# Keys and values in rings: the 24 V rows that two neighbouring tiles share are copied by ScalarE from one ring place to the next, for tiles 2 to 6 of each batch

## The chip, the cores and the metric

The program runs on one core of a Trainium2 chip. What counts is the device time of one execution in microseconds (us). The names of the engines are those of the profile: PE is TensorE, ACT is ScalarE, DVE is VectorE, POOL is GpSimd, SP is SyncE, which only issues DMAs here. A name with a q (SPq, ACTq) is that engine's instruction queue issuing a DMA.

## The reference

Chunked attention, then a soft mixture of experts, then a routed one. All data is float32.

```python
# attention: 4 batches, 8 heads, 768 tokens, head size 64, 8 memory tokens
for c in range(nc):                      # chunks of 32 queries
    l_start = max(0, c_start - 16)       # 16 tokens to the left
    r_end = min(S, c_end + 8)            # 8 tokens to the right
    k_full = np.concatenate([mem_k, k[:, :, l_start:r_end]], axis=2)
    v_full = np.concatenate([mem_v, v[:, :, l_start:r_end]], axis=2)
    scores = scale * np.matmul(q_c, k_full.transpose(0, 1, 3, 2))
    a = softmax(scores)
    out[:, :, c_start:c_end] = np.matmul(a, v_full)
# soft mixture: 3072 tokens, 512 wide, 8 experts x 4 slots, hidden 1024
logits = x @ phi; slot_input = softmax(logits, axis=0).T @ x
slot_out[e] = relu(slot_input[e] @ w1[e]) @ w2[e]
x = softmax(logits, axis=1) @ slot_out
# routed mixture: each token goes to one of 8 experts
out[mask] = gate * relu(x[mask] @ w1[e]) @ w2[e]
```

## The kernel before

**Tiles.** A tile is 96 query tokens (three chunks) of one batch with all 8 heads; a batch has 8 tiles, the program 32. A tile's keys and values are 120 token rows (96 with 16 to the left and 8 to the right) and 8 memory rows, 128 partitions in all. Neighbouring tiles overlap by 24 rows. The first tile of a batch starts at token 0 and the last ends at token 767, so there the overlap lies at other rows; for tiles 2 to 6 of a batch the first 24 rows of a tile are rows 96 to 119 of the tile to its left.

**Loads.** `k_in`, `q_in` and `v_in` are rings of four places each. SP runs through the tiles: in its round t it issues K (L399), the memory rows of K in the first two tiles of a batch (L401), Q (L403), and then V of tile t-4 (L410) with the memory rows of V (L412) for the first four tiles of a batch. A row of one head is 64 numbers, a packet of 256 bytes, so 96 rows are 768 packets and 120 rows are 960. K is loaded with 96 rows only, since ACT copies the overlap of the transposed keys inside SBUF (L1286). V was loaded with all 120. Before K of tile t SP waits until tile t-4 has been transposed (`kq_turned`); before V of tile t until tile t-4 has been weighted (`weighted`). `v_arrived[r]` counts the landings of place r, V and memory rows alike.

**The pipeline.** PE, ACT, DVE and POOL each run an instruction list written by hand, step j = 0 to 39, with the tiles staggered. On PE step j holds: transposes of the probabilities of tile j-4 (L625), scores of tile j-1 (L608; in every fourth step these two change places), transposes of K and Q of tile j (L644, L647), transposes of x of tile j-5 (L655), and last the product of V and probabilities of tile j-4 (L686), before which PE waits for V to have landed. On ACT step j holds: two copies of the transposed probabilities (L1258, L1263), the exponential of tile j-2 (L1251), copies of transposed Q and K of tile j (L1276, L1286, L1287), and last, once PE has done L686 of tile j-4, the copy of its result (L1298). POOL subtracts the row maximum (L549) and multiplies by the inverse row sum (L544). After four tiles come a few instructions more for the first router.

**Weights.** ACT issues one load of a 2 MB expert matrix every four steps (L1320, then L1326), after L1298, seven in all. When the last tiles of attention release their places, SP issues the other matrices in quarters (L434, each behind a wait for PE) and then whole (L499).

**After attention.** The first mixture (PE L750, L774), routing, then for half of the span the second mixture, in which PE is busy without a gap (L906, L916).

Of the kernel before, what the change touches and what calls it, by code (L numbers as in the profile page):

```python
# [24 lines left out]
def build(nc, q, k, v, mem_k, mem_v, phi, w1m, w2m, w_gate, w_ogate, w1, w2, out, rows_dram, g_dram):  # L25
    B, H, S, D = q.shape
    MEM = mem_k.shape[2]
    CHUNK, LEFT, RIGHT = 32, 16, 8
    CH = 3
    TQ = CH * CHUNK  # L30
# [21 lines left out]
    KQV = 4  # L52
# [30 lines left out]
    with ExitStack() as ctx:  # L83
# [3 lines left out]
        def sem(name):  # L87
            return ctx.enter_context(nc.semaphore(name))
# [128 lines left out]
        small_in = sem("small_in")  # L217
        kq_in = [sem(f"kq_in{i}") for i in range(KQV)]
        v_arrived = [sem(f"v_arrived{i}") for i in range(KQV)]
        kq_turned = sem("kq_turned")  # L220
        kt_copied = sem("kt_copied")
        qt_copied = sem("qt_copied")
# [116 lines left out]
        def k_rows(t):  # L339
# [2 lines left out]
            first = ends[t % TPB - 1] if t % TPB else 0  # L342
            return first, ends[t % TPB] - first

        def kq_landings(b, t):

            both = 48 if t % KQV < 2 else 32
            per_batch = both + 32 * (TPB // KQV - 1)
            uses = t // TPB * per_batch + both + t % TPB // KQV * 32
            return uses if b is None else b * per_batch + uses  # L350
# [9 lines left out]
        def quad_end(b, t):  # L360

            return live(b, t) and t % 4 == 3
# [9 lines left out]
        def heads(ap):  # L372
            return ap.rearrange("p (h d) -> p h d", h=H)
# [19 lines left out]
        def _(sp):  # L393
# [11 lines left out]
            def load_v(b, t, batch):  # L405

                r = t % KQV
                start = min(max(TQ * (t % TPB) - LEFT, 0), S - CTX)
                until(sp, weighted, b, t - KQV + 1)
                sp.dma_start(heads(v_in[0:CTX, r, :]), v_bs[batch, start:start + CTX]).then_inc(v_arrived[r], 16)  # L410
                if t % TPB < KQV:
                    sp.dma_start(heads(v_in[CTX:NK, r, :]), mv_bs[batch]).then_inc(v_arrived[r], 16)  # L412

# [182 lines left out]
        def _(pe):  # L596
# [32 lines left out]
            def step(b, j):  # L629
# [46 lines left out]
                if live(b, j - 4):  # L676

                    pe.wait_ge(v_arrived[(j - 4) % KQV], landings(b, j - 4, 16))
                    until(pe, pt_copied_low, b, j - 3)
                    until(pe, pt_copied_high, b, j - 3)  # L680
                    until(pe, xt_copied, b, j - 4)
# [561 lines left out]
        def _(act):  # L1243
# [21 lines left out]
            def step(b, j):  # L1265
# [27 lines left out]
                if live(b, j - 4):  # L1293

                    until(act, weighted, b, j - 3)
                    until(act, x_turned, b, j - 3 - XT)
                    quads_done(act, logit_made, b, j - 5)
                    sc.copy(x_t[:, (j - 4) % XT].rearrange("p c t -> p (c t)"), bank[6][:, 0:KD * TQ]).then_inc(xt_copied, 1)  # L1298
                if quad_end(b, j - 6):

                    g = (j - 6) // 4 if b is None else b * QPB + (j - 6) // 4
# [183 lines left out]
```

## Time and profile before

| | us |
|---|---|
| median of 3 runs | 486.86 (484.9 to 488.0) |
| profiled execution, its own time | 486.13 |
| its span, first to last instruction | 483.9 |
| PE busy | 447.3 (92%) |
| ACT busy | 269.1 (56%) |
| DVE busy | 214.4 (44%) |
| POOL busy | 179.6 (37%) |

The busy shares are means over stages that differ. Attention fills the span up to about 171 us, the first mixture with the routing lasts until about 243 us, and the rest is the second mixture. The line of the DMA shows 16 engines busy at 90% or more in nearly every slice up to 210 us, and at a tenth or less in most of the last 170 us. The line of bytes per second shows that the same busy engines move 160 to 280 GB/s during attention, and 420 GB/s after it.

### The profile page before, as it was taken

What the parts mean: (1) busy time and instruction counts of PE and PEld (TensorE: products, weight loads), DVE (VectorE), ACT (ScalarE), POOL (GpSimd) and SP (SyncE); (2) the same over time, 40 slices, a digit from 0 to 9 for tenths busy, and PEclk for the clock granted to TensorE, in tenths of its full rate; (3) what the DMA queues carried; (4) which work ended last, traced back from release to release, by engine and by line L of the source; (5) the groups of instructions that cost most, each with busy time, mean ns of one, the idle gap of its engine ahead of it and who ended that gap; (6) DMA issues with size and microseconds to landing.
All of it is one profiled execution on the core that took longest, in us unless ns stands there. A gap on an engine that the chain in (4) does not pass through costs nothing.

```text
span 483.9 us, 13207 instructions
## 1 busy us (share of the span) xinstructions
PE 447.3 (92%) x4708; PEld 251.3 (52%) x4709; DVE 214.4 (44%) x927; ACT 269.1 (56%) x465; POOL 179.6 (37%) x145
## 2 busy tenths in 40 slices
PE   4599999788999799998999999999999999999992
PEld 3488778577877653365554434443444344434430
DVE  2898988786899563019722112121212121212110
ACT  1587787575877520104164567665666566656540
POOL 2788887685888401000250122231223122101110
PEclk9999999998999999999999999999999999999998
DMA  9999999999999989999996976610011101000000
GB/s 156 192 262 234 234 275 215 225 272 184 281 241 273 372 315 336 427 429 420 420 389 221 407 279 238 219 45 25 23 46 39 31 23 46 32 34 22 24 0 0
DMA packets 98618, 95.63 MB, mean 198 GB/s; under 512 B 86664, under 2 KB 87096, under 8 KB 95896
## 3 DMA queue, kind: packets, MB, share of 16 engines
q1 hardware_dynamic: 93544, 73.18, 55.4%
q10 hardware_dynamic: 1792, 14.88, 8.2%
q0 software_dynamic: 3248, 7.14, 4.2%
q8 instruction: 19, 0.31, 0.3%
q14 instruction: 15, 0.12, 0.1%
HBM read 88.49 MB, written 7.74 MB: 199 GB/s over the span
## 4 chain that ended last, share of the span: by engine, by line
PE 66%; DVE 11%; SPq 10%; issue 4%; DMA 3%; POOL 3%; ACT 1%; DVEq 0%; ACTq 0%; POOLq 0%
PE bank L906 40%; PE bank L886 6%; DVE arena L1034 3%; PE bank L774 3%; SPq L410 3%; SPq L412 3%; SPq L399 2%; DMA arena<-in_mem_v_dram 2%; PE bank L625 2%; DVE row_sum L1053 2%; PE bank L831 2%; PE bank L686 2%; PE bank L608 2%; PE bank L703 1%; PE bank L750 1%
## 5 line engine op out<-in xcount | busy, mean ns | idle before, releaser
L916 PE MATMUL bank<-arena 128*64 128x512 f32 x448 | 196.5, 595 | 0.0
L906 PE MATMUL bank<-arena 128*64 (+1 forms) x448 | 196.5, 595 | 0.0
L906 PEld LDWEIGHTS bank<-arena 128*64 128x64 f32 x448 | 59.7, 137 | 119.9 <-issue 119.5
L1165 DVE TENSOR_SCALAR arena<-bank 128x256 f32<-128x256 f32 x112 | 39.7, 417 | 168.3 <-PE bank L886 96.4
L578 POOL DMA_INDIRECT out_dram<-arena,tok_sorted x28 | 28.3, 1010 | 177.0 <-ACT arena L1373 177.0
L549 POOL TENSOR_TENSOR arena<-arena,row_max 96x1024 f32<-96x1024 f32 x32 | 60.6, 1893 | 21.7 <-DVE row_max L1034 21.6
L544 POOL TENSOR_TENSOR arena<-arena,row_inv 96x1024 f32<-96x1024 f32 x32 | 60.6, 1894 | 17.5 <-DVE row_inv L1022 17.5
L1034 DVE CUSTOM_DVE_ANT_0 arena<-bank,masks 96x128 f32<-96x128 f32 x256 | 56.5, 282 | 15.0 <-issue 15.0
L1373 ACT ACTIVATE arena<-bank,gate_sorted 128x512 f32<-128x512 f32 x28 | 19.2, 687 | 75.3 <-PE bank L916 75.1
L916 PEld LDWEIGHTS bank<-arena 128*64 128x64 f32 x448 | 59.8, 137 | 0.0
L1393 ACT COPY arena<-arena 128x2048 f32 x27 | 51.3, 1898 | 3.2 <-DVE half_expert L1204 2.3
L1398 ACT COPY arena<-arena 128x2048 f32 x27 | 51.2, 1895 | 0.5 <-issue 0.4
L572 POOL DMA_INDIRECT arena<-rows_scratch,row_sorted x27 | 26.2, 970 | 61.8 <-DVE row_sorted L1193 53.9
L608 PE MATMUL bank<-arena 64*96 64x128 f32 x512 | 37.6, 288 | 5.6 <-ACT arena L1287 3.7
L1251 ACT ACTIVATE arena<-arena 96x1024 f32<-96x1024 f32 x32 | 34.0, 1062 | 12.7 <-POOL arena L549 12.5
L1053 DVE TENSOR_REDUCE row_sum<-arena 96x8 f32<-96x1024 f32 x32 | 38.6, 1206 | 0.7 <-ACT arena L1251 0.7
L608 PEld LDWEIGHTS bank<-arena 64*96 64x96 f32 x512 | 30.5, 167 | 14.2 <-ACT arena L1287 6.6
L686 PE MATMUL bank<-shared,arena 128*64 128x96 f32 x512 | 28.2, 252 | 8.6 <-DMA arena<-in_mem_v_dram 2.8
L625 PE MATMUL bank<-ident,arena 96*128 96x96 f32 x256 | 28.7, 256 | 1.7 <-DVE hid_rows_a L1059 1.0
L686 PEld LDWEIGHTS bank<-shared,arena 128*64 128x64 f32 x512 | 22.3, 137 | 14.6 <-issue 6.9
L625 PEld LDWEIGHTS bank<-ident,arena 96*128 96x128 f32 x256 | 22.8, 143 | 6.1 <-DVE hid_rows_a L1059 1.3
L1298 ACT COPY token_side<-bank 128x384 f32<-128x384 f32 x32 | 15.3, 478 | 18.1 <-PE bank L686 17.7
(189 smaller groups left out, 546.5 us busy)
## 6 DMA issues: line engine op xcount, KB each, us to landing
arena<-in_moe_w_dram SPq DMA_DIRECT2D x18, 2048.0 KB, 9.9
arena<-in_moe_w_dram ACTq DMA_DIRECT2D x7, 2048.0 KB, 9.4
arena<-in_moe_w_dram SPq DMA_DIRECT2D x24, 512.0 KB, 7.7
arena<-in_v_dram SPq DMA_DIRECT2D x32, 240.0 KB
arena<-in_q_dram SPq DMA_DIRECT2D x31, 192.0 KB, 5.0
arena<-in_k_dram SPq DMA_DIRECT2D x20, 192.0 KB, 4.5
arena<-in_moe_w_dram SPq DMA_DIRECT2D x2, 1024.0 KB, 9.2
arena<-in_k_dram SPq DMA_DIRECT2D x4, 240.0 KB
```

The lines of the kernel that those rows point to most:

```text
L544: g.tensor_tensor(probs[:, t % 4], probs[:, t % 4], row_inv[:, t % 2, :].unsqueeze(2).to_broadcast([TQ, H, NK]), ALU.mult).then_inc(p_norm ...
L549: g.tensor_tensor(probs[:, t % 4], probs[:, t % 4], row_max[:, t % 2, :].unsqueeze(2).to_broadcast([TQ, H, NK]), ALU.subtract).then_inc(sh ...
L608: ins = mm(bank[2 + h % 2][0:TQ, (h // 2) * NK:(h // 2 + 1) * NK], q_t[lo:lo + D, (j - 1) % 2, h // 2, :], k_t[lo:lo + D, (j - 1) % 2, h / ...
L625: ins = nc.tensor.transpose(bank[4 + h // 4][:, (h % 4) * TQ:(h % 4 + 1) * TQ], probs[:, (j - 4) % 4, h, :], ident[0:TQ, 0:TQ])
L686: ins = mm(bank[6][lo:lo + D, (h // 2) * TQ:(h // 2 + 1) * TQ], v_in[:, (j - 4) % KQV, h * D:(h + 1) * D], p_t[:, (j - 4) % 2, h, :], star ...
L906: mm(bank[4 + par][0:HR, :], h_t[:, par, lo:lo + HR], w2_all[:, bass.ds(at_w2 * SEG + f * DM, DM)], start=(f == 0), stop=(f == KF - 1))
L916: ins = mm(bank[4 + par][HR:TR, :], h_t[:, par, lo + HR:lo + TR], w, start=(f == 0), stop=(f == KF - 1))
L1034: ins = vec.tensor_tensor_reduce(out=probs[:, (j - 1) % 4, h, :], in0=bank[2 + h % 2][0:TQ, (h // 2) * NK:(h // 2 + 1) * NK], in1=masks[:, ...
L1053: vec.tensor_reduce(row_sum[:, j % 2, :], probs[:, (j - 2) % 4], AX.X, ALU.add).then_inc(row_summed, 1)
L1165: ins = vec.tensor_scalar(h_t[:, j % 2, 2 * r * 128:(2 * r + 2) * 128].rearrange("p (c a t) -> p a c t", c=2, a=2), bank[r][:, j % 2 * 256 ...
L1393: sc.copy(w2_second[j % 2][:, 0:SEG // 2], w2_all[:, bass.ds(e * SEG, SEG // 2)]).then_inc(second_low, 1)
L1398: sc.copy(w2_second[j % 2][:, SEG // 2:SEG], w2_all[:, bass.ds(e * SEG + SEG // 2, SEG // 2)]).then_inc(second_high, 1)
```

## The change

V of tiles 2 to 6 of a batch is loaded with its last 96 rows only. The 24 rows before them are copied inside SBUF by ACT from the place of the tile to the left: partitions 96 to 119 of one ring place to partitions 0 to 23 of the next, 512 numbers each. There are 5 such tiles in a batch, 20 in all. The copy into tile j-2 stands in ACT's step j behind L1298 and ahead of the weight load of that step. It waits for V of tile j-3 to have landed, and for tile j-6, the former content of the place, to have been weighted. PE waits, before it weights tile j-4, for the copy out of that tile's place into the next (`v_kept`), which ACT's step j-1 holds.

```diff
+        v_kept = sem("v_kept")
...
+        def v_shared(t):
+
+            return LEFT + RIGHT if 2 <= t % TPB < TPB - 1 else 0
+
+        def v_copies(b, t):
+
+            count = t // TPB * (TPB - 3) + min(max(t % TPB - 1, 0), TPB - 3)
+            return count if b is None else b * (TPB - 3) + count
...
-                sp.dma_start(heads(v_in[0:CTX, r, :]), v_bs[batch, start:start + CTX]).then_inc(v_arrived[r], 16)
+                kept = v_shared(t)
+                sp.dma_start(heads(v_in[kept:CTX, r, :]), v_bs[batch, start + kept:start + CTX]).then_inc(v_arrived[r], 16)
...
                     pe.wait_ge(v_arrived[(j - 4) % KQV], landings(b, j - 4, 16))
+                    if live(b, j - 3) and v_shared(j - 3):
+
+                        pe.wait_ge(v_kept, v_copies(b, j - 3))
...
+                if live(b, j - 2) and v_shared(j - 2):
+
+                    kept = v_shared(j - 2)
+                    act.wait_ge(v_arrived[(j - 3) % KQV], landings(b, j - 3, 16))
+                    until(act, weighted, b, j - 5)
+                    sc.copy(v_in[0:kept, (j - 2) % KQV, :], v_in[TQ:TQ + kept, (j - 3) % KQV, :]).then_inc(v_kept, 1)
```

ACT in the loop over batches, the end of the step that handles the tiles 0 and 6 of a batch and the start of the next, before:

```order
L1292 COPY shared<-bank 128x96 [waits logit_made]
L1298 COPY token_side<-bank 128x384 [waits logit_made,x_turned,weighted]
L1326 ISA
L1326 DMA arena<-in_moe_w_dram 128x4096
L1258 COPY shared<-bank 128x384 [waits weighted,p_turned]
L1263 COPY shared<-bank 128x384 [waits weighted,p_turned]
L1251 ACTIVATE arena<-arena 96x1024 [waits shifted]
```

And the same place with the change (its line numbers are higher):

```order
L1306 COPY shared<-bank 128x96 [waits logit_made]
L1312 COPY token_side<-bank 128x384 [waits logit_made,x_turned,weighted]
L1316 REGISTER_ALU
L1318 COPY arena<-arena 24x512 [waits weighted,v_arrived1]
L1346 ISA
L1346 DMA arena<-in_moe_w_dram 128x4096
L1272 COPY shared<-bank 128x384 [waits weighted,p_turned]
L1277 COPY shared<-bank 128x384 [waits weighted,p_turned]
L1265 ACTIVATE arena<-arena 96x1024 [waits shifted]
```

One copy with a wait for a landing stands ahead of the weight load, of both copies of probabilities and of the exponential.

SP in the same loop, the round that loads K and Q of tile 6 and V of tile 2 of a batch, before:

```order
L399 DMA arena<-in_k_dram 96x8x64
L403 ISA
L403 DMA arena<-in_q_dram 96x8x64
L410 ISA [waits weighted]
L410 DMA arena<-in_v_dram 120x8x64
L412 DMA arena<-in_mem_v_dram 8x8x64
```

With the change:

```order
L409 DMA arena<-in_k_dram 96x8x64
L413 ISA
L413 DMA arena<-in_q_dram 96x8x64
L421 DMA arena<-in_v_dram 96x8x64 [waits weighted]
L423 DMA arena<-in_mem_v_dram 8x8x64
```

The number and the order of SP's transfers stay; one of them in each of the 20 rounds is 24 rows shorter.

## Rows read from the trace of the kernel before

**Rows 1.** The page: busy time by engine, and the DMA's share in 40 slices.

```profile
PE 447.3 (92%) x4708; PEld 251.3 (52%) x4709; DVE 214.4 (44%) x927; ACT 269.1 (56%) x465; POOL 179.6 (37%) x145
...
DMA  9999999999999989999996976610011101000000
```

**Rows 2.** The chain of waits in attention: start us, us, what.

```profile
46.64 2.99 SPq L410
...
99.61 10.47 DMA arena<-in_mem_v_dram
110.12 0.88 PE bank L686 x16
...
123.07 1.05 PE bank L608 x16
```

**Rows 3.** Windows from one weight load of ACT to the next, four tiles each.

```profile
42.78:60.53 17.75, 17.46 (x251) 14.29 (x250) 16.51 (x89) 14.12 (x35) 14.92 (x9) 1.00 1.14 250
60.53:79.20 18.67, 17.88 (x253) 14.64 (x254) 17.03 (x89) 14.21 (x33) 15.29 (x9) 1.00 1.14 236
79.20:100.14 20.94, 17.59 (x251) 14.28 (x250) 16.59 (x89) 14.06 (x34) 14.92 (x9) 1.00 1.15 230
100.14:122.44 22.30, 19.45 (x253) 15.97 (x254) 16.58 (x89) 14.10 (x34) 15.11 (x9) 0.92 1.12 234
122.44:140.18 17.74, 17.45 (x251) 14.28 (x250) 16.47 (x89) 14.14 (x35) 14.88 (x9) 1.00 1.13 252
140.18:158.04 17.86, 16.96 (x243) 13.75 (x244) 16.61 (x89) 13.24 (x32) 15.02 (x9) 1.00 1.08 286
```

**Rows 4.** Timeline of PE: matmuls behind a wait for V, one after, and tile 27.

```profile
88.42 0.88 PE L686 MATMUL bank<-shared,arena 128*64 128x96 f32 x16 [2.17 <-DMA arena<-in_v_dram]
110.12 0.88 PE L686 MATMUL bank<-shared,arena 128*64 128x96 f32 x16 [2.78 <-DMA arena<-in_mem_v_dram]
...
112.27 2.03 PE L608 MATMUL bank<-arena 64*96 64x128 f32 x16
...
151.20 0.69 PEld L686 LDWEIGHTS bank<-shared,arena 128*64 128x64 f32 x16 [0.18 <-DMA arena<-in_mem_v_dram]
```

**Rows 5.** Windows without a weight load (the first two) and with one.

```profile
53.50:60.00 6.50, 6.21 (x105) 4.54 (x104) 6.45 (x35) 4.44 (x11) 5.58 (x4) 1.00 1.15 195
71.00:79.00 8.00, 7.82 (x121) 6.02 (x121) 7.57 (x39) 4.85 (x11) 6.53 (x4) 1.00 1.18 167
122.60:132.60 10.00, 10.00 (x134) 8.63 (x133) 8.78 (x51) 8.99 (x23) 8.06 (x6) 1.00 1.14 298
```

**Rows 6.** Timeline of SP's DMA issues: K of tiles 13, 14, 27 and 28.

```profile
53.24 0.34 SPq L399 DMA_DIRECT2D arena<-in_k_dram  x1
56.79 0.34 SPq L399 DMA_DIRECT2D arena<-in_k_dram  x1
...
119.28 1.19 SPq L399 DMA_DIRECT2D arena<-in_k_dram  x1
122.61 1.10 SPq L399 DMA_DIRECT2D arena<-in_k_dram  x1
```

**Rows 7.** Groups of ACT by shape from 20 to 170 us, and a long copy.

```profile
L1298 ACT COPY token_side<-bank 128x384 f32<-128x384 f32 x32 | 15.3, 478 | 18.1 <-PE bank L686 17.7
L1258 ACT COPY shared<-bank 128x384 f32<-128x384 f32 x32 | 15.2, 474 | 9.0 <-PE bank L625 9.0
...
L1286 ACT COPY arena<-arena 128x96 f32<-128x96 f32 x18 | 5.1, 283 | 0.0
...
L1393 ACT COPY arena<-arena 128x2048 f32 x27 | 51.3, 1898 | 3.2 <-DVE half_expert L1204 2.3
```

**Rows 8.** Timeline of ACT: the copy that ends its steps 21 and 30.

```profile
104.17 0.48 ACT L1298 COPY token_side<-bank 128x384 f32<-128x384 f32 x1 [0.34 <-PE bank L686]
...
148.23 0.48 ACT L1298 COPY token_side<-bank 128x384 f32<-128x384 f32 x1 [0.23 <-PE bank L686]
```

**Rows 9.** Waits of SP's queue from 40 to 175 us.

```profile
SPq L434 <- PE bank L696: 4.3, 2, 3.7
```

## The prediction

> **What bounds the kernel now.** The page comes first [rows 1]: PE is busy 92% of the span, which alone would say that shorter loads are worth nothing. The DMA line speaks against that for attention: all 16 engines are busy in every slice there. So I read the chain of waits next [rows 2]. From 46.64 us it runs through SP's issues (L410 first) with hardly a break, and ends in a landing of 10.47 us that releases PE at 110.12. A chain through SPq means that one issue could only start when the one before it was done: the queue, not an engine, sets the pace. The windows show what this costs [rows 3]. Four tiles take 17.75 us where nothing is late (17.74 and 17.86 in the last two windows), with PE busy for 17.46 of them. The windows at 60.53, 79.20 and 100.14 us take 18.67, 20.94 and 22.30. Their excess over 17.75 is 0.92 + 3.19 + 4.55 = **8.7 us**, and no more than that can be won in these stretches. PE's timeline names it [rows 4]: 2.17 us for V of tile 14, 2.78 us for V of tile 18, and matmuls of L608 that take 2.03 us soon after, where the same sixteen otherwise take 1.05 [rows 2], in a window whose granted clock is 0.92 on average [rows 3].
>
> Two rows tell what the queue's time consists of. Without a weight load the small packets move at 195 or 167 GB/s; with one the total is 298 [rows 5]. The weights take 2.1 MB of the 2.98 MB in those 10 us, so small packets get 0.9 MB instead of some 1.8. Every fourth step the queue loses about 5 us of its work to a weight load, and then it catches up. The last to be late is tile 27: its V comes at 151.20, and the row shows a wait of 0.18 us before PE's load of it, none before the matmuls [rows 4]. So after 110 us the queue has no spare time by 151 us either, though the windows there look clean. That matters: a pipeline that ran earlier in the middle would meet V of tile 27 too soon, unless the queue itself is earlier by as much.
>
> **The shorter loads.** Each of the 20 drops 192 packets of 256 bytes, 49,152 bytes. At 195 GB/s that is 0.25 us, at 167 GB/s 0.29 us [rows 5]. An upper bound: 120 rows cannot be dealt evenly to 16 engines, 96 can. If whole rows are dealt, the busiest engine has at least 8 rows, 64 packets, before, and 6 rows, 48 packets, after. One engine moves 195,000 / 256 / 16 = 47.6 packets in a us, so 16 packets fewer are 0.34 us. I take 0.30, between these ends. Of the 20 loads those count that SP issues while the queue is behind, from the first weight load at 25 us to tile 27: V of tiles 4 to 6, 10 to 14, 18 to 22, 26 and 27, 15 loads. 15 x 0.30 = **4.5 us** (3.8 to 5.1).
>
> Two rules of the Trainium skill bear on this. "DMA: Bandwidth & Descriptors", in its section on why a DMA increments its semaphore by 16, says that a load from SP runs on the largest number of engines, up to 16, that divides its row count: 15 for 120 rows, 16 for 96. By it the upper bound of 0.34 holds and the sum is 5.1; no row here shows how rows are dealt. The same page, in its specifications, gives a DMA about 2 us fixed plus bytes at 436 GB/s, which would make the dropped bytes worth 0.11 us; the trace's 195 GB/s for these loads disagrees, and the measurement decides, but the rule is kept as a rival.
>
> The number of transfers does not change. Were that the pace, nothing would be won. K of tile 13 to K of tile 14 is 3.55 us for four transfers, K of tile 27 to K of tile 28 is 3.33 us for three [rows 6]: a quarter fewer transfers, 3% fewer packets, and 6% less time. Packets explain it better.
>
> **The copy on ACT.** 96 numbers a partition take 283 ns and 2048 take 1898 [rows 7], so 512 take 283 + 416 x 0.827 = 627 ns. Twenty are 12.5 us of ACT. Its idle time before L1298 and L1258 is 18.1 + 9.0 us over 32 steps [rows 7], 0.85 us a step, so the copy fits: cost nothing while PE is what ACT waits for. If that cover were gone, the copies would cost their 0.63 us each, 12.5 us in all.
>
> **The new wait.** PE needs V of tile j-4 at the end of its step j. ACT now needs it at the end of its step j-1, one step earlier (17.75 / 4 = 4.4 us), for tiles 1 to 5 of a batch. Behind the waiting copy stand the weight load, both copies of probabilities (for which PE waits before L686) and the exponential (for which DVE waits). For tile 18 ACT would be there at 104.17 + 0.48 = 104.65, while it landed at 110.12 [rows 4, 8]: 5.5 us of waiting as things stand. For tile 27 it would be there at 148.71, and V came by 151.20: 2.5 us. PE waited for tile 18 anyway, so this is not added to its wait. What is added is the work between landing and L686: the copy, 0.63, and L1258 and L1263, 0.47 us each [rows 7], that now come after it and overlap a little, together about **1.4 us**. It is paid once, at the last place where the queue is late (tile 27), since the queue keeps its own timetable: a delay at an earlier place only gives it lead. PE's wait on `v_kept` adds nothing, the copy being a step older. Lower bound 0, if V comes in time; upper bound a whole step, 4.4 us, if ACT's list cannot catch up.
>
> **After attention.** SP's weight loads there are issued behind waits for PE, one of which alone shows 4.3 us [rows 9]. They start earlier by what attention ends earlier, so the gain is carried to the end.
>
> **Sum.** -4.5 + 1.4 = **-3.1 us**. The profiled execution took 486.13 and would take 483.0; the median, 0.73 above it, goes from 486.86 to **483.8**. With the bounds of both terms, -5.1 + 0 and -3.8 + 4.4, the case spans 481.8 to 487.5.
>
> **Rivals.**
> - *The queue's gain is larger and the wait is free.* With V one to two us earlier ACT finds it landed at most places, all 17 loads from tile 4 to tile 29 count at 0.34, 5.8 us; and if PE is not stopped at tile 18, its clock does not fall (2.03 us against 1.05 for L608) and all of the 8.7 us is in reach. Result -5.0 to -8.7, so 478.2 to 481.9. For it: the excess is there, and ACT's weight load moves behind the copy, so that it starts later against V of tile 18. Against: tile 27. Chance 0.30.
> - *The wait takes more than the loads give* (slower). ACT stops a step early behind each weight load, and the exponential stops with it, so DVE and POOL, at 16.5 and 15 of 17.75 us, cannot make it up. It decides where V lands later than about 1.5 us after the end of L1298, as at tile 18. Price: a step, 4.4, and 1.4 for the copies behind it, 5.8, less 0 to 4.5 from the loads: +1.3 to +5.8, so 488.2 to 492.7. Against: SP's timetable does not depend on ACT except through the ring. Chance 0.12.
> - *The loads give next to nothing.* If only 0.11 us a load is won, 15 x 0.11 = 1.7 and the 1.4 of the wait cancel. The time is then 486.6, between 485.5 and 488. By the fixed cost in the skill's page it would be this one; the trace's slow small packets speak against it. Chance 0.08.
>
> The forecast keeps 0.50.
>
> **The numbers.** One per cent, 4.9 us, is about what a measurement of this kernel tells from no change: below 482.0 is faster, above 491.7 slower. Faster gets nearly all of the first rival and a little of the forecast, 0.30. Slower gets half of the second, 0.06. Same keeps 0.64. The range leaves out the far part of the first rival, where most of the 8.7 us would have to come back, and the upper half of the second with a little of it below: 479.8 to 488.5.
>
> **What would show it.** Right: packets on q1 fewer by 3,840; in the windows of four tiles the excess shrinks from 8.7 to about 5.6 us; ACT has waits for V landings in place of PE's; windows without late V stay at 17.75. Wrong on the loads: the distance between SP's K issues for tiles 13 and 14 stays 3.55. Wrong on the wait: L1251 of ACT is preceded by long idle time and DVE waits for it. What would make the prediction wrong: V of tile 27 landing early enough to free the pipeline, or a weight load that now falls at a worse moment.

## The result, and the profile after

The changed kernel takes **485.06 us** at the median of its runs (480.85 to 490.21), the kernel before 487.33 on the same chip (484.9 to 490.9). The ratio is 0.9934, with a 95% interval of 0.9908 to 0.9959: 3.2 us less (2.0 to 4.5), inside the one per cent that I had called no change. Every ratio in this document leaves out the slow executions, those over 1.5% above the fastest of their kernel, while the medians hold all, so a ratio isn't the quotient of two medians. The forecast was -3.1 us and 483.8 us. Later pairs on two other chips gave 0.9946 (0.9908 to 0.9983) and 0.9944 (0.9908 to 0.9980).

The profiled execution of the changed kernel took 489.96 us (span 487.8) and lies well above its median: its first tile was late, and it waited longer for weights behind attention (both below). I therefore set a profile of the same kernel on another chip (span 482.6, the run after_third) beside it, and no reading of the gain rests on the first one alone.

The page of the changed kernel: busy time by engine, the DMA's share in 40 slices, and queue 1 with packets, MB and its share of 16 engines.

```profile
PE 451.8 (93%) x4708; PEld 255.2 (52%) x4709; DVE 214.1 (44%) x927; ACT 279.9 (57%) x485; POOL 179.8 (37%) x145
...
DMA  9979999999999987999996978601010101010000
...
q1 hardware_dynamic: 89724, 72.20, 53.1%
```

Against [rows 1] ACT has 20 instructions more and 10.8 us more. Queue 1, SP's, moved 93,544 packets before and 89,724 now: 3,820 fewer, where 3,840 were forecast. DMA is still busy in nearly every slice of attention, as before.

Six windows of four tiles each, from one weight load of ACT to the next. The columns are those of [rows 3]: length in us, busy time of PE, PE's weight loads, DVE, ACT and POOL with their counts, granted clock of PE, DMA share, GB/s.

```profile
46.44:64.19 17.75, 17.45 (x251) 14.28 (x250) 16.50 (x89) 14.69 (x35) 14.91 (x9) 1.00 1.13 243
64.19:82.66 18.47, 17.89 (x253) 14.65 (x254) 17.07 (x90) 16.08 (x38) 15.55 (x9) 1.00 1.13 242
82.66:100.40 17.74, 17.45 (x251) 14.27 (x250) 16.16 (x88) 14.69 (x36) 14.54 (x9) 1.00 1.12 249
100.40:120.41 20.01, 17.96 (x253) 14.68 (x254) 16.98 (x89) 16.21 (x38) 15.33 (x9) 1.00 1.13 246
120.41:138.15 17.74, 17.45 (x251) 14.28 (x250) 16.34 (x89) 14.68 (x36) 14.75 (x9) 1.00 1.08 248
138.15:157.04 18.89, 17.02 (x243) 13.77 (x244) 16.70 (x89) 15.26 (x35) 15.02 (x9) 1.00 1.09 278
```

The excess over 17.75 is now 0.72 + 2.26 + 1.14 = 4.1 us, where it was 8.7 [rows 3] and 5.6 was forecast. But it stands elsewhere. The window that took 20.94 us is clean at 17.74. The last one, clean before at 17.86, now has 1.1 us of excess. The clock of the window around 110 us is 1.00, where it was 0.92. That is this execution, and not the kernel: in the profile of after_again, the same kernel, the clock fell there as before the change:

```profile
100.07:121.99 21.92, 19.45 (x253) 15.45 (x253) 17.07 (x89) 16.20 (x38) 15.63 (x9) 0.92 1.04 238
```

What ends the wait around 110 us in the first profile, in the timeline of ACT (start us, us, what, idle time before it and its releaser):

```profile
111.84 0.61 ACT L1318 COPY arena<-arena 24x512 f32<-24x512 f32 x1 [2.48 <-DMA arena<-in_mem_v_dram]
112.37 0.25 ACT L1333 COPY shared<-bank 96x128 f32<-96x128 f32 x1
112.53 0.46 ACT L1272 COPY shared<-bank 128x384 f32<-128x384 f32 x1
112.90 0.46 ACT L1277 COPY shared<-bank 128x384 f32<-128x384 f32 x1
113.38 1.06 ACT L1265 ACTIVATE arena<-arena 96x1024 f32<-96x1024 f32 x1
```

And in the timeline of PE:

```profile
113.56 0.88 PE L700 MATMUL bank<-shared,arena 128*64 128x96 f32 x16 [1.69 <-ACT shared L1277]
```

ACT stands for 2.48 us before the new copy, for a landing. Both copies of probabilities follow it, and 1.69 us of PE's idle time end with the second. L700 is L686 of before: the wait of 2.78 us for V [rows 4] has become one for ACT. The chain of waits (start us, us, what) puts the same pieces in a row:

```profile
102.17 9.65 DMA arena<-in_mem_v_dram
...
112.62 0.37 ACT shared L1272
112.99 0.38 ACT shared L1277
113.56 0.88 PE bank L700 x16
```

From the end of the landing, 111.82, to L700 are 1.74 us. That is the work which the prediction put at 1.4 (a copy of 0.63 and two of 0.47 that overlap).

The waits from 20 to 175 us (total us, times, longest):

```profile
ACT arena L1318 <- DMA arena<-in_mem_v_dram: 4.2, 2, 2.5
ACT arena L1318 <- DMA arena<-in_v_dram: 1.2, 1, 1.2
PE bank L700 <- ACT shared L1277: 4.7, 4, 1.7
```

So it is not one place but three, at 78.31, 111.84 and 148.88 us. ACT issues its seven weight loads at 28.93, 46.78, 64.50, 82.98, 100.70, 120.73 and 138.45 us: the three waits stand behind the third, the fifth and the seventh. The schedule says why it is every second one. Those loads stand in the step of ACT that copies the result of a batch's tile 0, and the next four steps hold the copies into tiles 3 to 6 (the first load stands so, too, but nothing is late behind it). The loads between them stand in the step of tile 4, and the next three steps hold no copy and so no early wait.

Not all of PE's 4.7 us belong to the early wait: late_copy_2, below, which has none, shows 1.4 us in the same row. What is left is 3.3 us. The exponential behind the copy comes late too, and DVE waits for it longer. From the pages, before and changed:

```profile
L1053 DVE TENSOR_REDUCE row_sum<-arena 96x8 f32<-96x1024 f32 x32 | 38.6, 1206 | 0.7 <-ACT arena L1251 0.7
```

```profile
L1067 DVE TENSOR_REDUCE row_sum<-arena 96x8 f32<-96x1024 f32 x32 | 38.6, 1206 | 3.7 <-ACT arena L1265 3.7
```

And SP's queue from 28 to 165 us, first before and then changed:

```profile
SPq L410 <- PE bank L686: 3.0, 2, 1.6
```

```profile
SPq L421 <- PE bank L700: 7.0, 4, 2.4
SPq L445 <- PE bank L636: 6.7, 3, 3.4
```

SP now waits 7.0 us, not 3.0, for PE to give a place of V free. A step of the prediction turns on this, below.

**Where the profiled execution lost time.** Its span is 3.9 us longer than that of before. I split both at ACT's result copy (L1298, now L1312), whose start marks a tile. Up to tile 0 it took 28.92 us against 25.25, +3.7. From tile 0 to tile 31 it took 137.7 against 142.0, -4.3. Behind tile 31 it took 321.2 against 316.7, +4.6. The start is told by PE's timeline, first before, then changed:

```profile
13.24 1.12 PE L608 MATMUL bank<-arena 64*96 64x128 f32 x16 [1.15 <-ACT arena L1287]
```

```profile
13.39 2.02 PE L619 MATMUL bank<-arena 64*96 64x128 f32 x16 [1.15 <-ACT arena L1301]
22.62 2.02 PE L619 MATMUL bank<-arena 64*96 64x128 f32 x16 [1.12 <-ACT arena L1301]
```

The same sixteen matmuls took twice as long up to 24 us, ahead of the first changed copy at 29.4. The other profiles, of all kernels, reach tile 0 between 26.2 and 28.8 us. before_again, the kernel before, reaches it at 28.82 with the same groups at 2.02 us: the start varies between executions, and the change has no part in it. Behind attention the waits over the whole span show what is late:

```profile
PE bank L788 <- DMA arena<-in_moe_w_dram: 3.0, 2, 1.5
PE bank L845 <- DMA arena<-in_moe_w_dram: 1.7, 2, 1.2
```

Together 4.7 us; before, the one such wait of PE was 0.3 us. In after_third they are 0.7 and 0.2 us, and in before_again 1.8 together. The three parts of after_third are 27.8 us up to tile 0, 137.3 to tile 31, and 317.4 behind it.

### The profile page after: what moved, and what is told of

Its sections match the earlier page's. It is cut to its first block, busy times and chain, and to the rows that moved or that the text cites. A ratio compares the mean times of both kernels' runs of the same rounds, so it can differ in the third digit from the quotient of the medians.

```text
span 487.8 us, 13263 instructions
## 1 busy us (share of the span) xinstructions
PE 451.8 (93%) x4708; PEld 255.2 (52%) x4709; DVE 214.1 (44%) x927; ACT 279.9 (57%) x485; POOL 179.8 (37%) x145
## 3 DMA queue, kind: packets, MB, share of 16 engines
q1 hardware_dynamic: 89724, 72.20, 53.1%
## 4 chain that ended last, share of the span: by engine, by line
PE 64%; DMA 16%; SPq 7%; ACT 3%; issue 3%; POOL 3%; DVE 2%; ACTq 0%; POOLq 0%; DVEq 0%
PE bank L920 39%; DMA arena<-in_moe_w_dram 9%; PE bank L900 6%; DMA arena<-in_mem_v_dram 4%; PE bank L619 3%; PE bank L845 2%; SPq L423 2%; PE bank L700 2%; PE bank L636 2%; SPq L421 2%; SPq L413 2%; DMA arena<-in_v_dram 2%; PE bank L655 1%; PE bank L871 1%; PE bank L717 1%
## 5 line engine op out<-in xcount | busy, mean ns | idle before, releaser
L1179 DVE TENSOR_SCALAR arena<-bank 128x256 f32<-128x256 f32 x112 | 39.7, 416 | 169.2 <-PE bank L900 97.3
L560 POOL TENSOR_TENSOR arena<-arena,row_max 96x1024 f32<-96x1024 f32 x32 | 60.6, 1895 | 19.4 <-DVE row_max L1048 19.4
L619 PE MATMUL bank<-arena 64*96 64x128 f32 x512 | 39.4, 298 | 4.5 <-ACT arena L1301 4.4
L619 PEld LDWEIGHTS bank<-arena 64*96 64x96 f32 x512 | 32.0, 174 | 13.3 <-ACT arena L1301 6.5
L700 PE MATMUL bank<-shared,arena 128*64 128x96 f32 x512 | 28.9, 256 | 5.3 <-ACT shared L1277 4.7
L636 PE MATMUL bank<-ident,arena 96*128 96x96 f32 x256 | 28.8, 257 | 1.9 <-DVE hid_rows_a L1073 1.2
L700 PEld LDWEIGHTS bank<-shared,arena 128*64 128x64 f32 x512 | 22.9, 139 | 11.1 <-issue 10.1
L655 PE MATMUL bank<-ident,arena 96*128 96x96 f32 (+2 forms) x128 | 19.2, 278 | 6.3 <-DMA arena<-in_mem_k_dram 6.0
```

The lines of the kernel that those rows point to most:

```text
L560: g.tensor_tensor(probs[:, t % 4], probs[:, t % 4], row_max[:, t % 2, :].unsqueeze(2).to_broadcast([TQ, H, NK]), ALU.subtract).then_inc(sh ...
L619: ins = mm(bank[2 + h % 2][0:TQ, (h // 2) * NK:(h // 2 + 1) * NK], q_t[lo:lo + D, (j - 1) % 2, h // 2, :], k_t[lo:lo + D, (j - 1) % 2, h / ...
L636: ins = nc.tensor.transpose(bank[4 + h // 4][:, (h % 4) * TQ:(h % 4 + 1) * TQ], probs[:, (j - 4) % 4, h, :], ident[0:TQ, 0:TQ])
L700: ins = mm(bank[6][lo:lo + D, (h // 2) * TQ:(h // 2 + 1) * TQ], v_in[:, (j - 4) % KQV, h * D:(h + 1) * D], p_t[:, (j - 4) % 2, h, :], star ...
L1179: ins = vec.tensor_scalar(h_t[:, j % 2, 2 * r * 128:(2 * r + 2) * 128].rearrange("p (c a t) -> p a c t", c=2, a=2), bank[r][:, j % 2 * 256 ...
```

## The experiments

All ran on one core, in three groups on three chips, each beside the kernel before on its chip. Medians of different groups are not compared (the second chip was slower, mostly behind attention: 325 us there in before_again, rows104 and rows112, against 317 to 319); ratios are. "Us against before" is the ratio's distance from 1 times the median of before in that group.

| run | group | us, median | ratio (95%) | us against before |
|---|---|---|---|---|
| after_again | 1 | 486.16 | 0.9946 (0.9908 to 0.9983) | -2.6 (-4.5 to -0.8) |
| copy_only | 1 | 489.99 | 1.0039 (0.9998 to 1.0081) | +1.9 (-0.1 to +4.0) |
| short_only | 1 | 482.75 | 0.9892 (0.9859 to 0.9925) | -5.3 (-6.9 to -3.7) |
| late_copy | 1 | 483.73 | 0.9916 (0.9877 to 0.9955) | -4.1 (-6.0 to -2.2) |
| before_again | 2 | 495.38 | 1.0034 (0.9986 to 1.0082) | +1.7 (-0.7 to +4.1) |
| rows104 | 2 | 492.77 | 0.9985 (0.9932 to 1.0038) | -0.7 (-3.4 to +1.9) |
| rows112 | 2 | 491.99 | 0.9957 (0.9906 to 1.0008) | -2.1 (-4.7 to +0.4) |
| late_copy_quarters | 2 | 502.01 | 1.0213 (1.014 to 1.0286) | +10.6 (+6.9 to +14.2) |
| after_third | 3 | 484.88 | 0.9944 (0.9908 to 0.998) | -2.7 (-4.5 to -1.0) |
| wait_only | 3 | 488.59 | 1.0032 (0.9991 to 1.0074) | +1.6 (-0.4 to +3.6) |
| late_copy_only | 3 | 490.46 | 1.0029 (0.9987 to 1.0070) | +1.4 (-0.6 to +3.4) |
| late_copy_2 | 3 | 481.49 | 0.9878 (0.9826 to 0.9930) | -6.0 (-8.5 to -3.4) |

The median of before was 488.35, 495.83 and 488.28 us. before_again is the kernel before itself, compared with its own runs as any other. It came out at 1.0034 with 1 inside its interval: a tie looks like this. Where two versions are compared below, it is by the last column, within a group.

### The changed kernel once more (after_again), no edit

> The changed kernel once more, for another profiled execution. Theory A (shorter loads pay in attention, the gain is carried to the end): attention from the result copy of tile 0 to that of tile 28 takes 128 us as in the first profile of this kernel (132.8 before), and the total is 3 to 5 us below the kernel before. Theory B (attention gives the gain, the stream of expert matrices behind it takes part of it back): attention the same 128, but PE waits 2 to 5 us for matrices in the first mixture, where the kernel before waits under 1, and the total is 1 to 3 us below.

The gain repeats at 2.6 us. Tiles 0 to 28 take 129.9 us, more than the 128 expected. In its profile the windows behind the third to the sixth weight load are 19.32, 17.75, 21.92 and 17.75 us: again the excess stands behind the third and the fifth, but not behind the seventh this time (17.96). In the long one PE waited 2.47 us for ACT, and the clock fell to 0.92. One profile is no measure of such a window.

### The copy and the wait, with full loads (copy_only)

```diff
-                kept = v_shared(t)
-                sp.dma_start(heads(v_in[kept:CTX, r, :]), v_bs[batch, start + kept:start + CTX]).then_inc(v_arrived[r], 16)
+                sp.dma_start(heads(v_in[0:CTX, r, :]), v_bs[batch, start:start + CTX]).then_inc(v_arrived[r], 16)
...
-                    sc.copy(v_in[0:kept, (j - 2) % KQV, :], v_in[TQ:TQ + kept, (j - 3) % KQV, :]).then_inc(v_kept, 1)
+                    sc.copy(scrap[:, :], v_in[TQ:TQ + kept, (j - 3) % KQV, :]).then_inc(v_kept, 1)
```

> V is loaded with all 120 rows again; ACT makes the same 20 copies with the same wait for the landing of the left tile, but into unused memory. Cost of copy and wait without the shorter loads. By my forecast 1.4 us slower than the kernel before (0 to 4.4). Rival (the wait is free): within 0.5 us of it. Rival (the wait takes a whole step): 4 to 6 us slower.

+1.9 us, its interval just touching zero, so a cost is likely but not proven. The profile has the same waits, longer. From 40 to 165 us:

```profile
ACT arena L1318 <- DMA arena<-in_mem_v_dram: 6.5, 3, 3.1
PE bank L700 <- ACT shared L1277: 5.1, 3, 2.6
```

Behind the wait of PE that ends at 75.67 the clock falls; the same four tiles in one window:

```profile
62.00:84.00 22.00, 19.38 (x253) 15.22 (x252) 16.97 (x89) 16.43 (x38) 15.53 (x9) 0.92 1.11 235
```

PE's busy time for the four tiles is 19.38 us, where it is 17.89 at a clock of 1.00: a wait of 2.6 us cost another 1.5 in a lower granted clock. The window at 100.14 us before the change had the same mark [rows 3]. The early wait is not needed for it: late_copy_only, below, which has none, shows a window like it behind a wait of 2.40 us for Q.

### The short loads alone (short_only)

Here the 24 rows of V are neither loaded nor copied, and PE reads what the place held. It is so in 18 of the 20 tiles: tiles 2 and 3 of the first batch, where the places hold nothing yet, load all 120 rows.

```diff
-                kept = v_shared(t)
+                kept = v_shared(t) if b is not None or t >= KQV else 0
...
-                if live(b, j - 2) and v_shared(j - 2):
...
-                    sc.copy(v_in[0:kept, (j - 2) % KQV, :], v_in[TQ:TQ + kept, (j - 3) % KQV, :]).then_inc(v_kept, 1)
...
-                        pe.wait_ge(v_kept, v_copies(b, j - 3))
```

> V is loaded with 96 rows in tiles 2 to 6 of a batch (all 120 in tiles 2 and 3 of the first batch), nothing is copied and nothing waits for a copy, so the first 24 rows of V are those of an older tile there. The loads' gain alone: by my sum 4.5 us less than the kernel before (3.8 to 5.1), attention from tile 0 to tile 28 at 128 us or less. If only the bytes at full rate count (0.11 us a load): under 2 us. By theory B attention gains 4.5 us or more and the total less than 3.

-5.3 us (-6.9 to -3.7). The loads alone bring the whole gain and, by the middle values, more: -5.3 beside -2.6 in the same group. Tiles 0 to 28 take 125.1 us (132.8 and 129.1 in the two profiles of before), and the stretch behind tile 31 takes 318.6, as in the others, so the wrong values of V don't show there. Over 18 loads it is 0.29 us each, over the 15 that the prediction counted (all among the 18) 0.35. The distance between SP's issues for K of tile 26 and K of tile 27, in which V of tile 22 is shortened, is 2.38 us here; full loads have 3.29 to 3.44.

### The same copy one step later (late_copy, late_copy_2)

The copy into a tile moves from ACT's step j-2 to j-3, one step nearer to its use, and ahead of ACT's result copy. It then reads a V that PE needs in the same step anyway. So that the source isn't overwritten meanwhile, SP waits, in place of PE's weighting, for ACT's result copy (`xt_copied`), which stands behind the new copy.

```diff
-                until(sp, weighted, b, t - KQV + 1)
+                until(sp, xt_copied, b, t - KQV + 1)
...
-                    if live(b, j - 3) and v_shared(j - 3):
-                        pe.wait_ge(v_kept, v_copies(b, j - 3))
+                    if live(b, j - 4) and v_shared(j - 4):
+                        pe.wait_ge(v_kept, v_copies(b, j - 4))
...
+                if live(b, j - 3) and v_shared(j - 3):
+                    kept = v_shared(j - 3)
+                    act.wait_ge(v_arrived[(j - 4) % KQV], landings(b, j - 4, 16))
+                    until(act, weighted, b, j - 6)
+                    sc.copy(v_in[0:kept, (j - 3) % KQV, :], v_in[TQ:TQ + kept, (j - 4) % KQV, :]).then_inc(v_kept, 1)
```

> The copy into tile j-3 stands in ACT's step j ahead of the result copy of tile j-4, so it waits for V of tile j-4, which PE needs in the same step anyway; SP's V loads wait for the result copy in place of the product. The shorter loads without the early wait. Theory A: 1.4 us less than the changed kernel, 4.5 less than the kernel before. If the early wait is free: the same as the changed kernel. By theory B attention is 1.4 us shorter than in the changed kernel and the total is not.

> late_copy once more, on a chip with the two above. Theory A: the changed kernel's gain and the cost of the wait together, 4 to 5 us below the kernel before, and 1 to 2 us below the changed kernel. Rival (no cost of the wait): the same as the changed kernel.

-4.1 and -6.0 us against before. In both groups that is below the changed kernel on the same chip, by 4.1 - 2.6 = 1.5 and 6.0 - 2.7 = 3.3 us. Each pair of intervals overlaps, the second one barely; that both groups and the windows below point the same way is what the reading rests on. So a good part of the price is the step in which the wait stands, not the copy. Beside the short loads alone, the late copy stands 5.3 - 4.1 = 1.2 us higher, well inside both intervals.

The windows behind the third, fifth and seventh weight load, in the changed kernel (after_third):

```profile
63.10:81.46 18.36, 17.89 (x253) 14.68 (x254) 16.98 (x89) 16.21 (x37) 15.33 (x9) 1.00 1.12 247
99.20:118.62 19.42, 17.89 (x253) 14.68 (x254) 16.98 (x89) 16.21 (x37) 15.32 (x9) 1.00 1.14 249
136.37:155.60 19.23, 17.10 (x243) 13.78 (x244) 16.69 (x89) 15.25 (x35) 15.02 (x9) 1.00 1.07 274
```

and in late_copy_2:

```profile
63.91:82.03 18.12, 17.82 (x253) 14.65 (x254) 16.75 (x89) 16.22 (x38) 15.20 (x9) 1.00 1.02 238
99.77:117.89 18.12, 17.82 (x253) 14.65 (x254) 16.75 (x89) 16.22 (x38) 15.20 (x9) 1.00 1.18 260
135.62:153.48 17.86, 16.96 (x243) 13.75 (x244) 16.61 (x89) 15.24 (x35) 15.03 (x9) 1.00 1.09 282
```

PE's busy time differs by 0.07 to 0.14 us, the windows by 0.24, 1.30 and 1.37, together 2.9 us. In late_copy_2 neither PE nor ACT waits for a landing in attention from tile 0 on. This excess is the price of the early wait in this pair of profiles, and it agrees with the 3.3 us of the times. It also corrects a premise: the first two of these windows take 18.12 us with nothing late, since PE has 0.37 us more work in them than in a window of 17.75.

### The wait alone, and the late copy alone (wait_only, late_copy_only)

wait_only has full loads, ACT's early wait and no copy; late_copy_only is late_copy with full loads and a copy that nobody reads. The lines in which ACT's list differs, the first against the changed kernel, the second against late_copy:

```diff
-                    until(act, weighted, b, j - 5)
-                    sc.copy(v_in[0:kept, (j - 2) % KQV, :], v_in[TQ:TQ + kept, (j - 3) % KQV, :]).then_inc(v_kept, 1)
```

```diff
-                    sc.copy(v_in[0:kept, (j - 3) % KQV, :], v_in[TQ:TQ + kept, (j - 4) % KQV, :]).then_inc(v_kept, 1)
+                    sc.copy(scrap[:, j % TPB, :], v_in[TQ:TQ + kept, (j - 4) % KQV, :]).then_inc(v_kept, 1)
```

> V is loaded with all 120 rows and nothing is copied; ACT only waits, where the copy stood, for V of the left tile to land. Theory A (the early wait itself is the cost that copy_only showed): 1.5 to 2 us slower than the kernel before. Rival (ACT's 20 copies of 0.62 us are the cost): within 0.5 us of the kernel before.

> V is loaded with all 120 rows; ACT makes the 20 copies in late_copy's place, with late_copy's waits, but into unused memory. The copies without the early wait and without the shorter loads. Theory A: within 0.5 us of the kernel before. Rival (the copies cost): 1.5 to 2 us slower, up to 12 if nothing covers them.

+1.6 and +1.4 us, each with zero inside its interval, beside +1.9 for both at the early place. How the price divides between wait and copy where the loads are full can't be read from these three. By the last column late_copy_only is no cheaper than wait_only, against what I had expected (within 0.5 us of before).

In the profile of late_copy_only PE waits 2.40 us for Q before its matmuls at 75.62, and the clock falls in that window:

```profile
63.20:85.00 21.80, 19.40 (x255) 15.26 (x252) 17.03 (x89) 16.57 (x37) 15.44 (x9) 0.92 1.02 214
```

In wait_only ACT waits up to 3.86 us for a landing, no wait of PE is longer than 1.43, and no stretch of attention has a lower clock.

### The changed kernel a third time (after_third), no edit

> The changed kernel on the same chip as late_copy: 2.5 to 3.2 us below the kernel before, as in both comparisons so far, and attention from tile 0 to tile 28 at 128 to 130 us with ACT waiting for landings in two or three places.

-2.7 us. It pays at the same three places, also in the profile without the late start.

### The kernel before against itself (before_again), no edit

> The kernel before, for a second profiled execution. Its time against itself: within 2 us. Theory A (a gain in attention is carried to the end): attention from tile 0 to tile 28 near 132.8 us again, and the stretch behind attention 317 to 319 us as in the five others. Theory B (a shorter attention gets part of its gain taken back by the expert matrices): the stretch behind attention is 316.7 again, with PE waiting 0.3 us for matrices, against 317.7 to 321.2 in the changed kernels.

Its profile has none of the long waits for V that [rows 4] show, and no fallen clock; there PE waits for Q behind each of the last five weight loads (0.59 to 1.59 us). So which of SP's transfers is caught late varies between executions or chips; that one is, behind a weight load, holds in both profiles of before. Tiles 0 to 28 take 129.1 us here and 132.8 in the first profile: single profiles of one kernel lie 3.7 us apart, as much as the whole change.

### How many rows are dropped (rows104, rows112)

late_copy with 16 rows copied and 104 loaded, and with 8 copied and 112 loaded:

```diff
-            return LEFT + RIGHT if 2 <= t % TPB < TPB - 1 else 0
+            return LEFT if 2 <= t % TPB < TPB - 1 else 0
```

(and RIGHT for 112 rows)

> As late_copy, but only 16 of the shared rows are copied: V is loaded with 104 rows in tiles 2 to 6, 128 packets fewer than 120 rows, two thirds of what late_copy drops. If packets are dealt evenly: two thirds of late_copy's gain, 2.7 us below the kernel before, attention from tile 0 to tile 28 at 129 us. If whole rows are dealt to a number of engines that divides the row count (120 = 15 x 8, 104 = 13 x 8), the busiest engine has 64 packets as before: no gain, attention at 132 to 133 us, total within 1 us of the kernel before.

> As late_copy, but only 8 of the shared rows are copied: V is loaded with 112 rows (16 x 7), 64 packets fewer than 120 rows, a third of what late_copy drops. Evenly dealt packets: 1.4 us below the kernel before, less than rows104 gains. Whole rows dealt by a divisor: 56 packets on the busiest engine in place of 64, half of late_copy's step to 48, so about 2 us below the kernel before and more than rows104 gains, though more is loaded.

104 rows gave -0.7 us (-3.4 to +1.9), 112 rows -2.1 (-4.7 to +0.4). By dropped bytes, 104 rows should have brought two thirds of late_copy's gain (-4.1 and -6.0 on the other chips) and 112 rows one third. The order came out the other way about, the one that the rule on row counts in the Trainium skill's "DMA: Bandwidth & Descriptors" (why a DMA increments its semaphore by 16) gives: 13, 16 and 16 engines for 104, 112 and 96 rows, 15 for 120, so 8, 7, 6 and 8 rows an engine. No run proves it: the intervals overlap, and tiles 0 to 28 took 127.86 and 127.81 us in the two profiles. SP's round from K of tile 26 to K of tile 27, which holds one of the shortened loads, takes 3.29 us with 104 rows and 3.25 with 112, against 3.31 with 120 in before_again on the same chip: 104 rows save nothing there, as the rule would have it, but 112 rows save hardly more. It stays open.

### The weight loads in quarters (late_copy_quarters)

late_copy, with ACT's load of 2 MB every fourth step replaced by one of 512 KB in every step.

```diff
-                    if (j - LAG) % (TPB // EARLY) == 0:
-                        e = b * EARLY + (j - LAG) // (TPB // EARLY) + 1
-                        act.dma_start(arena[:, bass.ds(e * SEG, SEG)].rearrange("p (k n) -> p k n", k=KD),
-                                      w1m[bass.ds(e, 1)].rearrange("e (p k) n -> p (e k) n", p=128)).then_inc(early_in, 16)
+                    i = (j - LAG) % KD
+                    e = b * EARLY + (j - LAG) // KD + 1
+                    act.dma_start(arena[:, bass.ds(e * SEG + i * F, F)],
+                                  w1m[bass.ds(e, 1)].rearrange("e (p k) n -> p (e k) n", p=128)[:, i, :]).then_inc(early_in, 16)
```

> late_copy, with ACT's 2 MB loads in the loop cut into four of 512 KB, one in each step. The DMA work is the same, its bursts are gone. If the late landings come from the bursts, no load of V, K or Q is late, attention goes to the 124 to 125 us of a pipeline that never waits, and the total is 1 to 3 us below late_copy. If they come from the sum of the work, attention stays at 127 us and the total with late_copy's.

I had expected 1 to 3 us less than late_copy. It is 10.6 us more than the kernel before (6.9 to 14.2), the only version whose interval lies wholly above it. The queues from 60 to 140 us, with packets, MB and share of 16 engines, and the weight loads with their landing times. In late_copy_2:

```profile
q1 hardware_dynamic: 43656, 10.94, 85.3%
q10 hardware_dynamic: 621, 9.13, 29.1%
...
arena<-in_moe_w_dram ACTq DMA_DIRECT2D x5, 2048.0 KB, 9.2
arena<-in_q_dram SPq DMA_DIRECT2D x17, 192.0 KB, 4.5
```

In late_copy_quarters:

```profile
q1 hardware_dynamic: 35995, 9.02, 77.0%
q10 hardware_dynamic: 2325, 8.47, 39.7%
...
arena<-in_moe_w_dram ACTq DMA_DIRECT2D x16, 512.0 KB, 7.2
arena<-in_q_dram SPq DMA_DIRECT2D x15, 192.0 KB, 6.8
```

late_copy_2 ran on another chip. The profile of rows104, on this chip, with loads of 2 MB and V of 104 rows, says the same:

```profile
q1 hardware_dynamic: 42927, 10.77, 81.2%
q10 hardware_dynamic: 594, 8.68, 28.9%
...
arena<-in_q_dram SPq DMA_DIRECT2D x18, 192.0 KB, 4.8
```

ACT's queue carried 0.66 MB less than in late_copy_2 and held the engines for longer. Its packets are 3.6 KB on average (8.47 MB / 2325) where they were 14.7 KB, and a MB takes 39.7 / 8.47 = 4.7% of the engines' time in place of 3.2% (3.3% in rows104). Queue 1 moved 1.9 MB less in the same 80 us, and the median landing of Q takes 6.8 us in place of 4.5 (4.8 in rows104). The loss is in attention: tiles 0 to 28 take 138.3 us, against 127.9 in rows104. Part of it is a lower granted clock, 0.96 on average from 60 to 140 us where the other two have 1.00. I had spread the load in time and, with the same edit, cut each partition's run of memory to a quarter. The two are not told apart by this run, so it says nothing against spreading a load whose packets stay long.

## Why the prediction was right, and where not

- **The shorter loads, -4.5 us (3.8 to 5.1): right.** Alone they gave -5.3 us (-6.9 to -3.7), an interval that holds the forecast. What can lie on top is the clock, which the prediction kept for its first rival: 0.92 in the window around 110 us before, 1.00 throughout attention in short_only, late_copy and late_copy_2. In the changed kernel it is 1.00 in two profiles and falls in the third, and before_again has 1.00 with full loads, so how much of the -5.3 it is stays open. The rival that the loads give next to nothing (0.11 us each) is refuted: 15 x 0.11 = 1.7 us, or 2.0 for the 18 loads, is outside the interval. The formula behind it, about 2 us and bytes at 436 GB/s, stands in the Trainium skill's "DMA: Bandwidth & Descriptors" in the section on the anatomy of one DMA, fitted to DMAs that GpSimd issues, and not in its specifications; these loads are issued by SP.
- **The 8.7 us in reach were counted too high.** The prediction took 17.75 us for every window in which nothing is late. Behind the third and fifth load that is 18.12 (late_copy_2), so 8.7 - 0.37 - 0.37 = 8.0 us.
- **The sign to look for, K of tile 13 to K of tile 14, was ill chosen.** SP issues V of tile t-4 in its round t, so the load between those two is V of tile 9, the second of its batch, which the change leaves at 120 rows. It could not show the gain, and in the changed kernel a weight load falls in there too (9.16 us). A round that can is that of tile 26, with V of tile 22. In the timeline of SP's issues of the changed kernel:

```profile
114.14 0.61 SPq L409 DMA_DIRECT2D arena<-in_k_dram  x1
...
117.04 1.06 SPq L409 DMA_DIRECT2D arena<-in_k_dram  x1
```

  2.90 us. With full loads the five profiles (before, before_again, copy_only, wait_only, late_copy_only) have 3.29 to 3.44, with short loads the six of group 1 and 3 and of the result 2.38 to 3.02. So the round with a short load is 0.3 to 1.1 us shorter, at a constant number of transfers.
- **The copy, 0.627 us each: right in size, "nothing" not shown.** The trace of the changed kernel over 20 to 170 us, by shape:

```profile
L1312 ACT COPY token_side<-bank 128x384 f32<-128x384 f32 x32 | 15.4, 480 | 9.3 <-PE bank L700 8.4
...
L1318 ACT COPY arena<-arena 24x512 f32<-24x512 f32 x20 | 12.3, 616 | 5.9 <-DMA arena<-in_mem_v_dram 4.2 <-DMA arena<-in_v_dram 1.2
```

  It takes 0.616 us. ACT's idle time before its result copy fell from 18.1 [rows 7] to 9.3 us, so most of the copies lie in time in which ACT waited for PE, as argued. Whether all do stays open: the late copy stands 1.2 us above none at all, within the noise.
- **The new wait, 1.4 us "paid once": the step that failed.** The price at one place was right: ACT's wait, then copy, L1272 and L1277, 1.74 us from landing to L700, and 1.30 and 1.37 us in two of the windows of after_third. "Once" was wrong. The wait is met behind the third, fifth and seventh weight load (in after_again behind the first two of these), and moving it away brings 1.5 and 3.3 us in the times (0.24 + 1.30 + 1.37 = 2.9 in the windows). With the copy it costs 5.3 - 2.6 = 2.7 us in group 1, where 1.4 was forecast. I had argued that the queue keeps its own timetable, so that a delay of PE at an earlier place only gives it lead. It doesn't keep it: V of a tile may only be loaded once PE has weighted the tile that held its place. The 7.0 us that SP waits for that are not the mark of the early wait, since short_only has 9.6 us of the same row and late_copy_2 8.9 us for ACT's result copy. They show that with shorter loads the queue no longer runs behind all the time but waits for the engines between bursts. And no window is shorter than 17.74 us, so time lost at one place isn't made up at the next. That each delay is handed on in full is argued from these rows, not measured alone.
- **The sum was right by luck.** By the middle values both terms were too small, and the errors cancel: in group 1 the loads gave -5.3 for -4.5, wait and copy cost 2.7 for 1.4, and the changed kernel measured -3.2, -2.6 and -2.7 in three comparisons. Only the second error is seen in the traces, too; the first is inside its interval.
- **The sign "DVE waits for the exponential", set for "wrong on the wait", came in part:** DVE's wait for it rose from 0.7 to 3.7 us, with 0.8 in late_copy_2.
- **The rival "larger gain, free wait"** (-5.0 to -8.7 us) describes late_copy_2, 6.0 below before, and just misses late_copy, 4.1 below. Its condition, a free wait, is what moving the copy by a step made true. Its 5.8 us for the loads are inside the measured 3.7 to 6.9, as the forecast's 4.5 are.
- **The slower rival** (the wait takes more than the loads give) did not happen. With full loads something near it is likely: copy_only shows 6.5 us of waits of ACT and is 1.9 us slower (-0.1 to +4.0). With short loads the price stayed below the gain.
- **Carried to the end: yes.** The rival in the expectations is that what attention gains is lost behind it. From tile 31 to the end the profiles of groups 1 and 3 take 317.2 to 318.6 us, and the first profile of before 316.7, though tiles 0 to 28 take anything from 124.8 us (late_copy_2) to 134.6 (copy_only). The exception is the first profile of the changed kernel, 321.2, with its 4.7 us of waits for matrices. Whether the change makes such an execution likelier is open; the two further profiles, 318.4 and 317.4, don't speak for it.

The best version measured that computes the reference is late_copy: faster than before on both chips it ran on, and ahead of the changed kernel on both, by less than the intervals can settle in group 1.

## What to carry to other kernels

Where a DMA queue sets the pace, dropping bytes that are already on the chip pays about what the queue's own rate says (0.25 to 0.29 us a load by the rate, 0.29 measured, with 0.2 to 0.4 inside the interval). Place the instruction that replaces them where its input is waited for anyway: one step earlier, in the list of an engine on which others depend, it took 1.5 and 3.3 us out of gains of 4.1 and 6.0. Before a delay is counted "once", count the places where the wait stands behind a burst (here every second weight load), and look whether the queue waits for the delayed engine anywhere.

## What the hardware showed that I had not expected

- Cutting a load of 2 MB into four made its packets 3.6 KB in place of 14.7, its share of the DMA engines 4.7% a MB in place of 3.2%, and the kernel 2.1% slower (1.4 to 2.9) than before. The other queue's landings of 192 KB went from 4.5 to 6.8 us. The Trainium skill's "DMA: Bandwidth & Descriptors" (the rule in its section on bandwidth) advises transfers of at least 1 MiB. The trace agrees in direction, 2 MB against 512 KB, but the edit shortened the runs of memory too, and it can't say which of the two counted. It adds that another queue's landings slow down with it.
- PE's matmuls at the start ran at half their speed until about 12 us in one profile (1.12 us at 13.24) and past 22 us in others (2.02 at 22.62), with a granted clock of 1.00 from 12 to 24 us in both. The first tile came 3 us later in those, as much as the whole change, and in both kernels. What causes it is open.
- The long waits of PE and the granted clock (1.00 is the upper of its two levels): waits of 2.78 us (before), 2.47 (after_again), 2.61 (copy_only) and 2.40 (late_copy_only) were each followed by a window with 0.92 on average, and PE's busy time for the four tiles was 19.4 us in place of 17.9: 1.5 us on top of the wait. No such window follows the single waits of 1.35 to 1.69 us in the changed kernel, nor one of 2.17 in before [rows 4]. But behind two waits close together in copy_only, 1.28 and 1.59 us long and ending at 149 and 152 us, the clock was 0.50 from 152 to 156 us and 0.74 from 156 to 160. So a wait can cost more than its length, and its length alone doesn't tell whether it will.
